# Settled tokens chosen ahead of the last two row tiles: a reordering at the seam of two mixture-of-experts layers

## What is computed

```python
x = attention(q, k, v)         # 8 heads of 64; 4 sink tokens and a causal window of 128
# first MoE: 8 experts of 512 x 1024 and 1024 x 512, two experts per token
logits = x @ w_gate; noisy = logits + log1p(exp(x @ w_noise)) * noise
out[t] = sum over the two largest e of weight_e * (relu(x[t] @ w1[e]) @ w2[e])
# second MoE: one expert per token
logits = x @ w_gate2 + modality_bias[modality_id]
e = argmax(logits); out[t] = softmax(logits)[e] * (relu(x[t] @ w1[e]) @ w2[e])
```

## Time and profile before

| | us |
|---|---|
| median of three runs | 689.15 |
| lowest and highest of them | 684.98, 690.12 |
| the profiled execution, its own time | 686.28 |
| span of the profiled execution, first to last instruction | 684.3 |
| mean granted TensorE clock | 0.98 |

### The profile page before, as it was taken

One profiled execution on the slowest core, in us unless ns is written; L12 is line 12 of the kernel. 1 busy time (PEld: TensorE's weight loads), 2 busy tenths in 40 slices (PEclk: granted clock), 3 DMA queues, 4 the chain that ended last, 5 costly groups with the idle time before them and its releaser, 6 DMA issues.

```text
span 684.3 us, 11242 instructions
## 1 busy us (share of the span) xinstructions
PE 642.9 (94%) x3866; PEld 583.5 (85%) x3867; DVE 328.7 (48%) x681; ACT 275.7 (40%) x529; POOL 185.0 (27%) x199
## 2 busy tenths in 40 slices
PE   7989999899999999999999998998789999999981
PEld 6989999898999999999999998977667888788861
DVE  4566646586465527163452715537677222542210
ACT  5668866443344344252434423333416123522110
POOL 2500100127361623516152332101442121121010
PEclk9999999999999999999999999998999999999996
DMA  7877721354585546656463502606576211001000
GB/s 208 273 249 246 266 81 61 107 205 132 174 240 157 100 125 152 188 140 181 120 149 111 148 14 34 184 16 214 110 289 227 99 47 46 20 31 47 15 32 11
DMA packets 51089, 89.84 MB, mean 131 GB/s; under 512 B 7919, under 2 KB 14063, under 8 KB 51040
## 3 DMA queue, kind: packets, MB, share of 16 engines
q1 hardware_dynamic: 41872, 69.21, 30.2%
q0 software_dynamic: 9168, 19.97, 13.4%
HBM read 73.13 MB, written 17.02 MB: 132 GB/s over the span
## 4 chain that ended last, share of the span: by engine, by line
PE 81%; DVE 7%; DMA 4%; issue 3%; ACT 2%; SPq 1%; ACTq 0%; DVEq 0%; POOL 0%; POOLq 0%
PE banks L1055 6%; PE banks L1054 6%; PE banks L1073 6%; PE banks L994 5%; PE banks L993 5%; PE banks L996 5%; PE banks L798 5%; PE banks L826 4%; PE banks L1338 4%; PE banks L1339 4%; PE banks L1343 3%; PE banks L1366 3%; PE banks L1367 3%; PE banks L1370 3%; PE banks L810 2%
## 5 line engine op out<-in xcount | busy, mean ns | idle before, releaser
L1817 DVE TENSOR_TENSOR split<-stage,split 128x2048 fp32r<-128x2048 f32 x32 | 73.3, 2290 | 42.6 <-ACT split L1448 42.5
L993 PE MATMUL banks<-xTs,split 128*128 128x416 f32 (+1 forms) x256 | 88.7, 351 | 1.9 <-issue 1.9
L994 PE MATMUL banks<-xTs,split 128*128 128x416 f32 (+1 forms) x256 | 86.5, 342 | 0.0
L1054 PE MATMUL banks<-hTs,split 128*128 128x416 f32 x224 | 81.4, 363 | 0.0
L645 POOL DMA_INDIRECT x_moe<-rows,dst_idx x25 | 50.3, 2012 | 114.8 <-DVE rows L2267 112.6
L1055 PE MATMUL banks<-hTs,split 128*128 128x416 f32 x224 | 80.0, 357 | 0.0
L1583 ACT ACTIVATE hTs<-banks 128x416 fp32r<-128x416 f32 x56 | 29.0, 518 | 85.4 <-PE banks L996 85.4
L1448 ACT ACTIVATE split<-stage 128x2048 fp32r<-128x2048 f32 x32 | 60.9, 1907 | 0.8 <-DMA stage<-w1a 0.8
L1705 ACT ACTIVATE hTs<-banks 128x512 fp32r<-128x512 f32 x28 | 16.5, 597 | 105.3 <-PE banks L1353 105.3
L996 PE MATMUL banks<-xTs,split 128*128 128x416 f32 (+1 forms) x256 | 56.2, 340 | 0.0
L798 PE MATMUL banks<-k_sb,q_sb 128*128 128x260 f32 (+2 forms) x192 | 49.1, 380 | 3.8 <-DMA k_sb<-k_w 2.0
(11 more groups left out here) (371 smaller groups left out, 1311.1 us busy)
## 6 DMA issues: line engine op xcount, KB each, us to landing
stage<-w1a SPq DMA_DIRECT2D x16, 1024.0 KB, 7.9
stage<-w2a SPq DMA_DIRECT2D x16, 1024.0 KB, 5.5
k_sb<-k_w SPq DMA_DIRECT2D x12, 520.0 KB, 4.8
raw<-w1b SPq DMA_DIRECT2D x4, 1024.0 KB, 5.3
raw<-w2b SPq DMA_DIRECT2D x4, 1024.0 KB, 8.3
q_sb<-q_t SPq DMA_DIRECT2D x24, 128.0 KB, 3.1
x_attention<-rows SPq DMA_DIRECT2D x12, 256.0 KB, 6.1
split<-x_moe SPq DMA_DIRECT2D x12, 256.0 KB, 4.2
```

Source lines behind the costliest of these rows:

```text
L993: pe.matmul(psum, piece(slot, 0, o + c * FH), xTs[:, 0, c, 0:cols], start=(c == 0), stop=False)
L994: pe.matmul(psum, piece(slot, 1, o + c * FH), xTs[:, 0, c, 0:cols], start=False, stop=False)
L1054: pe.matmul(psum, piece(e % 2, 0, o), hTs[:, 0, c, 0:cols], start=(c == 0), stop=False)
L1817: dve.tensor_tensor(split_chunk(e % 2, 1, c), staged_chunk(e % 2, c), split_chunk(e % 2, 0, c).bitcast(F32), ALU.subtract).then_inc(low_do ...
```

## The change

No computation is added or removed. On VectorE `last_one_hot(2)` goes behind `x2_low(8)`, `last_one_hot(3)` behind `x2_low(9)`, and `sure_choice` ahead of `x2_low(10)` and `x2_low(11)`; `popular_low(0)` goes ahead of `popular_first` and `last_share`, `popular_low(1)` ahead of the final choice, `chosen_gate` ahead of `second_hots`, `second_sources` up to between the low parts of chunks 2 and 3, and `expert_order` down behind `h_low(0, 1)`. On PE `back(7, 2)` and `(3)` go behind `tx(0)`, and `codes2` ahead of `th(0, 1)`. On ScalarE `popular_high(0)` goes ahead of `y1_copy(7, 3)`, `popular_high(1)` ahead of `last_scale(0)`, and `x_high(0)` ahead of `last_scale(2)` and `(3)`. On SP chunks 2 and 3 wait for the gathers of tiles 0 and 1, and the next expert's chunks for the gather of tile 2. The wait of PE for the row list ahead of `back(7, 2)` goes, and its wait ahead of tile 2 is on `fresh_tiles` instead of `second_sources`, since the tile table is now written after the list.

```diff
@@ SP
                 if c == 2:
                     sp.wait_ge(y1, DC * E)
+                    for b in range(EARLY2):
+                        sp.wait_ge(gathered[b], 16)
...
             sp.wait_ge(last_added, 1)
+            sp.wait_ge(gathered[0], 32)
@@ PE
             last_to_tokens()
-            pe.wait_ge(early_src_ready, 2)
-            back(last, 2, banks[:, 3, :])
-            back(last, 3, banks[:, 4, :])
+
...
                 tx(0, 0, 1)
+                back(last, 2, banks[:, 3, :])
+                back(last, 3, banks[:, 4, :])
                 first(0, 0, 0, 1)
...
                 first(1, 1, 0, 1)
+                codes2()
                 th(0, 1)
-                codes2()
                 second(0, 0, 1)
                 slot_gates()
                 th(1, 0)
                 th(1, 1)
                 second(1, 0, 1)
-                pe.wait_ge(slots_ready[1], 1)
+                pe.wait_ge(fresh_ready[1], 1)
@@ ACT
                 turned_copy(2)
+                popular_high(0)
                 y1_copy(last, 3)
...
-                popular_high(0)
+                popular_high(1)
                 last_scale(0)
-                popular_high(1)
-                for k in range(1, SUBS):
-                    last_scale(k)
+                last_scale(1)
                 x_high(0)
+                last_scale(2)
+                last_scale(3)
                 popular_high(2)
@@ DVE
-                for t in range(TILES):
+                for t in range(TILES - 2):
                     x2_low(t)
+                    if t == 8:
+                        last_one_hot(2)
+                last_one_hot(3)
                 sure_choice()
-                last_one_hot(2)
+                x2_low(TILES - 2)
+                x2_low(TILES - 1)
                 popular_places()
                 popular_sources()
-                last_one_hot(3)
-                popular_first()
...
+                popular_low(0)
+                popular_first()
                 last_share()
-                popular_low(0)
+                popular_low(1)
                 late_scores()
...
                 x_low(0)
-                popular_low(1)
                 second_places()
                 x_low(1)
+                chosen_gate()
                 second_hots()
-                chosen_gate()
-                expert_order()
                 popular_low(2)
+                second_sources()
                 h_low(0, 0)
                 popular_low(3)
                 h_low(0, 1)
+                expert_order()
                 tile_owners()
-                second_sources()
                 fresh_tiles()
```

More of the change, by code:

```diff
@@ L2384, in first_layer, with popular_low @@
                 last_one_hot(1)
-                for t in range(TILES):
+                for t in range(TILES - 2):
                     x2_low(t)
+                    if t == 8:
+                        last_one_hot(2)
+                last_one_hot(3)
                 sure_choice()
-                last_one_hot(2)
+                x2_low(TILES - 2)
+                x2_low(TILES - 1)
                 popular_places()
                 popular_sources()
-                last_one_hot(3)
-                popular_first()
+            def popular_low(c):
+                dve.wait_ge(high_done[c], E + 1)
+                dve.tensor_tensor(split_chunk(1, 1, c), staged_chunk(1, c),
+                                  split_chunk(1, 0, c).bitcast(F32), ALU.subtract).then_inc(low_done[c], 1)
             def expert_phase():
@@ L2441, in step @@
                     y_copy(t - 1, 1 - b, went)
[L2443 to L2446, removed]
                 def second_weights(chunks):
```

## The result

| | before | after |
|---|---|---|
| median | 688.33 us (4 runs, 684.98 to 690.12) | 680.32 us (4 runs, 678.91 to 682.25) |
| ratio | | 0.9891, 95% interval 0.9845 to 0.9938 |
| ratio, measured again | | 0.9892, interval 0.9847 to 0.9936 (medians 693.28 and 685.30) |
| profiled span | 684.3 us | 678.7 us |

The ratios leave out executions more than 1.5% above the fastest of the same kernel; the medians are of all. The change makes the kernel faster, by less than 2%: the interval of the ratio is 0.6 to 1.6% of time saved. The forecast was 683.4 us with a range of 678.5 to 689.0, and 0.6% saved.

What follows compares the result with a forecast made beforehand. PE follows DVE from `last_share` on, so the start of `second(1)` decides. 686.28 - 5.5 + 1.3 = 682.1 us on the profiled execution, a gain of 4.2; mean 687.6 less that gain gives 683.4, range 678.5 to 689.

Steps and rivals of the forecast that it cites:

- Part 1: Settled tokens' choice on DVE: begins at 457.5 instead of 461.27; last `second1` ends at 468.1 instead of 473.0.
- Part 2: Chunk 0 and what follows: new PE wait of about 1.8 us; final choice at 476.95, 1.65 us earlier.
- Part 3: Tile 0 and ranks: `tx(0)` at 476.0 finds its rows, ranks out at 482.15; SP's wait worth almost nothing.
- Part 4: DVE from the places to `y_copy(0)`: `second(1)` starts at 503.4 against 508.48; gain so far 5.5 us.
- Part 5: PE's clock: new waits may bring half level; cost taken as 1.3 us, bounds 0 and 3.4.
- The first stretch: Half clock coming near 475 and going near 485: rest of `first(0, 0)` and the ranks take 1.2 us longer.
- The second stretch: Half clock coming at 503: `second(1)` at half speed for some 5 us, 2.2 us more.
- the same distance from there to the end: Sign of being right: from `second(1)`, at 503 to 505, to the end takes as long as before.
- the clock staying high: Rival: PE's clock stays high throughout, all 5.5 us gained, 682.1 us; chance 0.20.
- ScalarE's order: Rival: all from `y1_copy(7, 3)` waits for chunk 0, landing in 7 us, not 5.1; gain 2.3, 685.3; chance 0.20.
- The half level that holds on: Rival: many short waits keep PE's clock at half from 470 until `second(1)` is through; 689.6 us; chance 0.10.
- the rule that was weighed: DMA engines taking turns between queue rows: a gather would lose little beside a bulk load; trace's 8.2 against 3.3 us disagrees.

Runs made afterwards that it cites:

- clock_kept: The changed kernel with idle matmuls in PE's waits ahead of the last logits, `last_to_tokens` and `second(1)`; ratio to the kernel before 0.9926.
- choice_only: The kernel before with only `sure_choice` ahead of the last two row tiles and the one-hots moved; scores to `second(1)` 46.86 us, ratio 0.9892.
- mix: `choice_holds` plus `back(7, 2)` and `(3)` behind `tx(0)`, and `x_high(0)` ahead of `last_scale(2)` and `(3)`; scores to `second(1)` 47.75 us, ratio 0.9936.
- copy_first: The changed kernel with `y1_copy(7, 3)` put back ahead of `popular_high(0)` on ScalarE; scores to `second(1)` 47.87 us, ratio to the kernel before 0.9964.
- after_again: The changed kernel, not edited, timed again beside the kernel before; scores to `second(1)` 47.84 us, ratio 0.9892.
- no_holds: The changed kernel without SP's three waits on the gathers; scores to `second(1)` 47.41 us, ratio to the kernel before 0.9887.
- rest_only: The changed kernel with the old order of row tiles, `sure_choice` and one-hots; scores to `second(1)` 55.83 us, ratio to the kernel before 1.0057.
- rest_no_holds: `rest_only` without SP's three waits on the gathers; scores to `second(1)` 52.21 us, ratio to the kernel before 1.0005.
- choice_holds: `choice_only` plus SP's wait that keeps chunks 2 and 3 behind the gathers of tiles 0 and 1; scores to `second(1)` 47.46 us, ratio 0.9935.

## Why the prediction was right, point by point

The forecast of the time held, at 683.4 for 680.3, and so did the direction. The path through the seam was right, step by step. Between the medians lie 8.0 us where 4.2 were forecast, and the seam accounts for 3.1 to 4.8 of them. With 0.87 us added to the times after, for the earlier start of the seam, the steps stand as follows.

- *Part 1.* Choice at 457.5, measured 457.5. PE's 2.6 us wait and the half clock behind it gone: yes, `second1` ends at 468.0, forecast 468.1. The one-hots fit their gaps.
- *Part 2.* Chunk 0 turned from 468.2: 468.2. A new wait of PE of about 1.8 us: 1.80. Final choice at 476.95: 476.9.
- *Part 3.* `tx(0)` at 476.0: 476.0. The gather took 3.5 us to land, the near end of my bounds. The ranks were out at 482.6 instead of 482.15: `x_low(0)` started 0.4 us later than the bare durations gave, by the gaps between linked instructions, and the four matmuls behind it took a little longer after their wait.
- *Part 4.* `second_hots` done at 490.4 instead of 489.8. (In the sum of part 3, 482.15 + 3.4 gives 485.55 and not 485.3; nothing hangs on it, since `x_high(1)` came later.) `second_sources` took 0.5 us more than before, with GpSimd at its products beside it. The list of tile 2 came in time, though its gather left at 495.2, 1.4 us later than forecast: the list was ready at 494.5 instead of 493.4, and GpSimd was still at its products; nothing waited for it. `second(1)` at 504.5 instead of 503.4. The two rows of `second_sources`, of which the first (L2118 before) took 0.18 us:

```profile
493.09 0.51 DVE L2122 SCALAR_TENSOR_TENSOR src_idx<-shared 128x21 int32<-128x21 f32 x1
...
493.75 0.42 DVE L2124 TENSOR_SCALAR shared<-shared 128x21 f32<-128x21 f32 x1
```

- *Part 5.* Both low stretches came in the profiled execution, and only the first in the repetition. Measured to tile 2, the gain is 3.1 us in the first, and 4.5 or 4.8 in the second by which kernel before it is set against; the forecast was 5.5 less 1.3. The term was near the 1.6 and the 0 us that the clock cost in the two executions, but not for its reasons. The first stretch, which I took for the likelier to cost, came in both and cost next to nothing, as `clock_kept` shows at the ranks (25.2 us from the scores with a full clock, 25.35 and 25.15 without), where I had 1.2; the missing 1.1 us by `second(1)` are the small pieces of parts 3 and 4. The second stretch cost 1.6 where I had 2.2.

Two things in it were wrong all the same.

*What each part is worth.* The sum ran along one path and gave each part its segment. That path was right and the attribution was not. Part 2 says of the new wait on ScalarE, "What this buys: DVE's low part runs ... where DVE would have been idle". `choice_only` shows what it was set against: without parts 2 to 4 the final choice starts 3.5 us sooner, and the seam is 0.8 us shorter up to `second(1)` and as long up to tile 2. I had compared each step with the kernel before, never with the kernel that has only the step ahead of it. In the same way part 3 priced SP's waits at almost nothing, which holds (0.3 us), but the sentence that the late chunks "hold ScalarE's queue (...) no longer than PE needs" is true only of this kernel; with the late choice the waits cost 3.6 us, with the early one and the moves of `mix` 2.7 (47.75 against 45.09).

*The size of the whole.* The timed gain is 1.1% where I had 0.6%, the interval of which just takes in the seam's 3 to 5 us. I left the tail out of the sum as the same code. It is, and still differs by 1.6 us between executions, with one more half clock in the longer ones. The sign "the same distance from there to the end" came true, 175.1 us from `second(1)` for 175.8, but by luck: 0.9 us more up to tile 2 and 1.7 less behind it. What the medians gained beyond the seam comes from nothing that the prediction names.

Of the rivals, the clock staying high did not happen in the changed kernel; made to happen it was worth 1.6 us. ScalarE's order costs nothing by itself in the traces, and chunk 0 landed when forecast (468.2), not after 7 us; the timed ratio of `copy_first` leaves the order's price open. The half level that holds on came nowhere in the changed kernel; in `choice_only` it lasted 10 us and the distance was still shorter, so its price was overstated where DVE sets the pace. Two numbers of that rival do not fit the sum: the change would have lost from 8.4 us of low level beyond what the sum holds (twice its 4.2), not from 11, and the range's high end of 689 lies below the rival's own 689.6.

On the rule that was weighed: the gather of tile 0 took 3.5 us in the changed kernel, where chunk 1's load still ran for the first 2.9 of them, and 7.0 us in `choice_only` beside the loads of chunks 2 and 3. The Trainium skill, "DMA: Bandwidth & Descriptors", section "Queues, rings and completion order", says that each DMA engine takes turns between the queue rows that have work, packet by packet. The traces disagree with a reading of it by which the gather would lose little.

## What to carry to other kernels

When a change has several parts, price each against the kernel that has the others, not against the kernel before: here one part alone gave as much as the whole up to tile 2, and the rest cost 4.1 us up to `second(1)` when alone and 0.8 beside it. On an in-order engine that several chains share, put the work that releases others first and bulk work (weight parts) into the gaps that remain; holding a bulk load back to speed a small gather moves the wait to whoever stands queued behind that load. And where executions of the same code differ by 1%, measure from an event ahead of the change to one behind it: that distance repeated within 0.15 us, while the span wandered by several.

## What the runs showed of the hardware

- The clock fell to half behind a PE wait of 1.8 us between matmuls of 8 columns (at 470.5 us, after), and behind one of 1.8 us ahead of `second(1)` (504.5 us). The same wait of 1.8 us at that place stands in six profiles (after, `after_again`, `no_holds`, `copy_first`, `rest_only`, `rest_no_holds`): the clock fell in after and `no_holds` and stayed full in the other four. Low stretches in the seam lasted from 3 to 10 us.
- Chunk 3, held back by SP's wait, took 11.0 us in `choice_holds` (issued at about 473.5, there at 484.6), while the last expert's accumulating scatters ran, 10.4 in `after_again` and 7.6 in after; a chunk's load took 5.0 us at best (`clock_kept`; 5.1 in rows 8).
- Tile 0's gather took 3.4 to 3.9 us where SP held chunks 2 and 3 back (4.3 in `rest_only`), 6.6 to 7.0 beside them with the early choice, and 8.1 to 8.2 with the late one.
- About 160 us into the span an execution could lose 1.7 to 8.3 us to a wait of PE, with a half clock of 3 to 10 us during or behind it, in code that none of the kernels changed.
